# Attention inside a fused kernel: third and fourth group of transposes in one go, the fourth copy ahead of the scaling

## What is computed

```
B, H, S, D = 4, 8, 576, 64; window = 128
scores = scale * q @ k^T
scores = where(0 <= i - j < window, scores - slope_h * |i - j|, -1e9)
attn = exp(scores - max); attn = attn / (sum(attn) + 1e-9)
x = attn @ v                                   # heads side by side: B x S x 512
h = (x^T @ U @ V)^T;  u = x + h
x = u + relu(u @ w_ch1) @ w_ch2
h = relu(x @ w_in); split into u, v; v normalised, mixed over tokens by w_spatial, + b_spatial
out = (u * v) @ w_out
```

## Time and profile before

| | |
|---|---|
| median of 3 runs | 717.57 us (716.21 to 717.58) |
| the profiled execution | 718.08 us |
| its span, first to last instruction | 716.3 us |
| TensorE matmuls busy | 705.1 us, 98% |
| TensorE weight loads busy | 659.8 us, 92% |
| VectorE busy | 452.4 us, 63% |
| ScalarE busy | 339.0 us, 47% |
| GpSimd busy | 178.9 us, 25% |
| TensorE clock granted, mean | 0.998 of full |

### The profile page before, as it was taken

One profiled execution on the slowest core, in us unless ns is written; L12 is line 12 of the kernel. 1 busy time (PEld: TensorE's weight loads), 2 busy tenths in 40 slices (PEclk: granted clock), 3 DMA queues, 4 the chain that ended last, 5 costly groups with the idle time before them and its releaser, 6 DMA issues.

```text
span 716.3 us, 12975 instructions
## 1 busy us (share of the span) xinstructions
PE 705.1 (98%) x4624; PEld 659.8 (92%) x4624; DVE 452.4 (63%) x1032; ACT 339.0 (47%) x765; POOL 178.9 (25%) x183
## 2 busy tenths in 40 slices
PE   8999999999999999999999999999999999999998
PEld 5677777789999999999999999999898998998997
DVE  6979797898673274339868967976384354354341
ACT  5888788864352243234443444444352432432422
POOL 2498646510009807650050000000010100100100
PEclk9999999999999999999999999999999999999999
DMA  7659974055547856799276175468800100100101
GB/s 215 194 194 395 366 277 143 17 191 177 220 147 266 303 181 217 263 384 382 92 244 217 45 264 183 156 216 283 336 1 1 67 0 0 66 0 0 66 1 67
DMA packets 72145, 122.46 MB, mean 171 GB/s; under 512 B 4896, under 2 KB 43808, under 8 KB 71584
## 3 DMA queue, kind: packets, MB, share of 16 engines
q1 hardware_dynamic: 72096, 121.82, 49.1%
HBM read 74.29 MB, written 47.51 MB: 170 GB/s over the span
## 4 chain that ended last, share of the span: by engine, by line
PE 75%; DVE 4%; ACT 0%; issue 0%; DVEq 0%
PE bank L1917 8%; PE bank L1919 8%; PE bank L1918 8%; PE bank L1959 4%; PE bank L1961 4%; PE bank L1960 4%; PE wide L1959 3%; PE wide L1961 3%; PE wide L1960 3%; PE bank L2068 2%; PE bank L2070 2%; PE bank L2069 2%; PE bank L1884 2%; PE bank L1882 2%; PE bank L1883 2%; PE wide L1883 2%
## 5 line engine op out<-in xcount | busy, mean ns | idle before, releaser
L1917 PE MATMUL bank<-xs,w1s 128*128 128x384 f32 x336 | 113.0, 336 | 1.0 <-DVE tok L1442 0.8
L1919 PE MATMUL bank<-xs,w1s 128*128 128x384 f32 x336 | 112.3, 334 | 0.0
L1918 PE MATMUL bank<-xs,w1s 128*128 128x384 f32 x336 | 112.3, 334 | 0.0
L1075 ACT ACTIVATE rk<-tok 128x768 fp32r<-128x768 f32 x72 | 61.0, 849 | 71.3 <-PE bank L1961 32.4
L916 POOL TENSOR_TENSOR vl<-vr,vh 128x512 fp32r<-128x512 f32 x8 | 11.3, 1407 | 291.9 <-ACT vh L1200 291.9
L1053 ACT ACTIVATE sums_u<-bank 128x384 f32<-128x384 f32 x72 | 35.4, 491 | 88.7 <-PE bank L1919 88.5
L929 ACT ACTIVATE sc<-sc,mn 128x256 f32<-128x256 f32 (+1 forms) x144 | 67.0, 469 | 18.6 <-DVE mn L1260 18.4
L1959 PE MATMUL bank<-rk,w2q 128*128 128x384 f32 x208 | 69.9, 336 | 0.3 <-DVE rk L1464 0.3
L1960 PE MATMUL bank<-rk,w2q 128*128 128x384 f32 x208 | 69.5, 334 | 0.0
L1961 PE MATMUL bank<-rk,w2q 128*128 128x384 f32 x208 | 69.5, 334 | 0.0
L1917 PEld LDWEIGHTS bank<-xs,w1s 128*128 128x128 f32 x336 | 63.1, 188 | 2.7 <-issue 1.3
(11 more groups left out here) (212 smaller groups left out, 1822.1 us busy)
## 6 DMA issues: line engine op xcount, KB each, us to landing
r_scr<-tok SPq DMA_DIRECT2D x20, 768.0 KB, 3.9
tok<-r_scr SPq DMA_DIRECT2D x15, 768.0 KB, 7.1
w1raw<-w SPq DMA_DIRECT2D x32, 256.0 KB, 3.9
w2q<-w_scr SPq DMA_DIRECT2D x4, 2048.0 KB, 11.1
wc_scr<-wprep SPq DMA_DIRECT2D x12, 512.0 KB, 6.5
w_scr<-tok SPq DMA_DIRECT2D x11, 512.0 KB, 3.8
qkraw<-qk SPq DMA_DIRECT2D x16, 320.0 KB, 5.0
qkraw<-qk SPq DMA_DIRECT2D x16, 288.0 KB, 3.8
```

Of the source, the lines that this page charges most:

```text
L1075: act.activation(rk[:, n % RING, 0], raw(g, RAW_OF[m])[:, 2 * j:2 * j + 2, :], ACT.Relu if m <= 3 else ACT.Copy).then_inc(rk_hi, 1)
L1917: pe.matmul(o, wh, ah, start=(k == 0 and m in FRESH), stop=False, skip_group_check=True)
L1918: pe.matmul(o, wl, ah, start=False, stop=False, skip_group_check=True)
L1919: last = pe.matmul(o, wh, al, start=False, stop=(k == 1), skip_group_check=True)
```

## The change

On TensorE, in every pair step, the fourth group of transposes moves from behind the turning back of the earlier pair to directly behind the third group. On VectorE the copy of the fourth group moves from behind the scaling of the earlier pair to ahead of it. Nothing else changes: the same instructions with the same waits, in another order. TensorE's written-out tail stays as it was.

```diff
--- before.py
+++ after.py
@@ -1321,10 +1321,10 @@
                 score(b, i, range(0, AFTER_X))
                 if i == 2 and (whole or b >= 1):
                     lo_t(b - 1)
+                if one:
+                    keep_pt(*back(b, i, 1), 3)
                 if two:
                     normalise(*back(b, i, 2))
-                if one:
-                    keep_pt(*back(b, i, 1), 3)
                 score(b, i, range(AFTER_X, NT))
                 if whole or b >= ago:
                     add_u(b - ago, k, pt_ps)
@@ -1846,10 +1846,9 @@
                 scores_z(b, i)
                 if one:
                     turn(*back(b, i, 1), 2)
+                    turn(*back(b, i, 1), 3)
                 if two:
                     turn_back(*back(b, i, 2))
-                if one:
-                    turn(*back(b, i, 1), 3)
                 scores_y(b, i)
                 if two:
                     turn_x(*back(b, i, 2))
```

## The result

| | before | changed |
|---|---|---|
| median of 5 runs | 717.57 us (716.21 to 717.80) | 720.05 us (719.46 to 720.46) |
| span of the profiled execution | 716.3 us | 718.6 us |

The ratio is 1.0040 with a 95% interval of 1.0029 to 1.0052. The changed kernel is slower by 2.5 us; the forecast was 720.6, +3.0.

A forecast was written before the change was run, and what follows sets the result against it. TensorE was taken as the bound, its matmul row busy 705.1 of 716.3 us. Step losses 1.53 + 0.96 + 0.68 + 0.21 = 3.38, less 0.34 given back, made +3.0: 720.6 us, range 718.6 to 722.2.

The forecast's parts named there:

- the load of `qkraw`: In p = 6 (pair steps p = 4b + i) TensorE waits for this late load; up to 0.34 us given back.
- fourth pairs: p = 15, 11, 7, counted with p = 5: scaling 0.58 later less 0.40 slack, 0.17 us each, 0.68 for four.
- third pairs: p = 6, 10, 14: no slack, scaling 0.61 later, 0.10 back before the mixing; 0.51 us each, 1.53 for three.
- p = 3: Fourth pair step of batch 0: a loss of 0.21 us, lower bound 0.09.
- p = 2: Pair step of batch 0: its 0.3 us loss is taken by the next step's 1.71 wait for VectorE.
- p = 4: First pair step of batch 1: loss and the filled 0.20 us wait for `xt` cancel, 0.
- The slack: How late the scaled tile may come before TensorE's turn: 0.23 us in p = 12, 0.40 in p = 15, none in p = 14.
- Copy to scaling: VectorE, from the fourth copy's start to the scaling's start: 0.72 us taken, 0.60 as lower bound.
- First and second looped pairs: p = 8, 9, 12, 13: scaling 0.48 later less 0.23 slack, 0.24 us each, 0.96 for four.
- Only third pairs pay: Rival, attention stage: slack covers all other steps; about +1.0 us, 718.6; chance 0.15.
- Faster: Rival: the earlier copy releases TensorE sooner before each step's value products; -2.7 us, 714.9; chance 0.05.
- ScalarE caught: Rival: delayed `xh` and `tok` copies push ScalarE's exponentials in the last batch; +4.9 us, 722.5; chance 0.12.

## Why the prediction was right

The direction and the mechanism came out; the time was 0.5 us below the forecast. That the sum came so close is in part luck. Before the load of `qkraw` the forecast had 3.38, and the loss by the steps without that load was 3.09. But the fourth pairs were 0.68 too high, and third pairs (0.30), p = 3 (0.11) and p = 2 (0.06) too low; p = 4 was 0.14 too high. By its steps:

*Starting point.* Right. Time lost in TensorE's queue in attention is lost at the end: 2.38 at the stage's last turn, 2.3 in the span.

*The slack.* Right in its size in most steps. Two points of the fourth pairs confirm it: in p = 15 the scaled tile is 0.42 later against its score in the changed kernel and the turn loses 0.04; with the copy alone it is 0.96 later and the turn loses 0.58. Both leave 0.38, where the forecast had 0.40. The 0.23 is right for p = 9 and 13 but not for p = 12, from which it was worked out: there the scaled tile came 0.44 later and the turn lost 0.28, so the slack was 0.16 (p = 8 has 0.17). The forecast took 0.05 from VectorE's end to TensorE's turn, the value of p = 14; in p = 12 it is 0.12.

*Copy to scaling.* Mis-sized. I took 0.72 between their starts, from the pair L1301 and scaling, with 0.60 as the bound. The changed kernel has 0.61 in p = 4, 5, 7, 11, 15; the 0.77 and 0.78 in p = 8, 9, 12, 13 are turning back, which ends late. The copy alone shows 0.60 in these four too. In third pairs, however, the copy stands 0.72 behind L1301, and the scaling again 0.72 to 0.73 behind the copy (p = 14: 124.05, 124.77, 125.50). Each starts 0.03 or 0.04 after the end of the instruction ahead, where in p = 4, 5, 7, 11 and 15 the scaling starts 0.08 or 0.09 before the copy's end. So the 0.72 does not come with the scaling as follower, as the forecast had it; it comes with L1301, and reaches past the copy. What the Trainium skill says in VectorE: DVE Perf Modes, section The DRAIN you can't avoid, that a semaphore on each of a chain of copies adds nothing, agrees with the 0.60 to 0.61 behind the copy. What makes the two instructions behind L1301 wait 0.72 stays open. L1301 is the one of these whose operands start at partition 64 (`low` in the code); the others start at partition 0. No run here varied that.

*Third pairs.* Mechanism right, forecast 0.51 each, measured 0.60 to 0.62: the copy stands 0.72 behind L1301 and not 0.61. The 0.10 ahead of the mixing came back as foreseen. Three steps: 1.83 against 1.53.

*First and second looped pairs.* Forecast 0.24 each, measured 0.28, 0.22, 0.26, 0.21: 0.97 against 0.96. Of the sum's terms this is the closest, but two errors meet in it: the scaled tile came 0.43 to 0.45 later and not 0.48, and in p = 8 and 12 the slack was smaller. Bound by turning back (0.54 behind its last load, before and after), one of the two releasers the forecast named.

*Fourth pairs and p = 5.* Forecast 0.17 each, 0.68; measured 0.04 at the idle time and -0.04 to 0.04 from turn to turn. This is the term that was mis-sized most, the price of 0.72 taken for 0.60. The lower bound, 0.07, was nearer.

*The rest.* p = 3 0.32 (forecast 0.21). p = 4 gained 0.14 (forecast 0), with this row in place of the wait of the earlier trace rows:

```profile
36.71 0.55 PEld L1794 LDWEIGHTS wide<-ident,xt 128*128 128x128 f32 x5
```

p = 2 lost 0.20, of which 0.14 went in p = 3's wait; the forecast had all of it go there. The late `qkraw` took 0.2 in the profile (0.34 in the forecast), but as it moves between executions this term was no more than a guess.

*The rivals.* Only third pairs pay: wrong, the first and second looped pairs lose 0.97 beside them. Faster: the gap before the value products stayed at 0.16 with the copy long done; it isn't a wait for the copy. ScalarE caught: its wait for the scaled tile appears, but its delay stays inside its idle time, and the turns show no loss beyond VectorE's. The Trainium skill's Perfetto Trace Analysis, section Identifying the Most-Contended Engine, would have the most-contended engine optimised first. What that engine does was the same here (matmuls busy 705.1 and 704.7 us, weight loads 659.8 and 658.7), and 2.5 us were lost in what it waits for.

What the text had missed is the coupling that the halves show: TensorE's half needs VectorE's, else the mixing waits for the copy; VectorE's half without TensorE's costs three times the whole.

## What to carry to other kernels

When an order is changed in a queue, find the instruction whose result the busiest engine waits for, and compare its delay with the slack in each kind of step; a sum over kinds held here to 0.5 us, with single steps off by up to 0.2 both ways and some of that cancelling. Filling an engine's idle time ahead of such an instruction is only free up to the slack: 0.38 in fourth pairs, 0.16 to 0.23 in first and second, nothing in third. Two halves of a reordering on two engines have to be costed together.

## What the runs showed of the hardware that I had not expected

- Of several waits ahead of one VectorE instruction it matters which is met last: 0.54 us from the releasing engine's last load with two further waits behind it, at most 0.40 with the same wait last, in the first and second pairs of the looped batches; elsewhere 0.36 and at most 0.41.
- Behind a VectorE copy of 0.69 us the next instruction starts after 0.60 to 0.61 us, before the copy's end. With L1301 just ahead of the copy, both the copy and the scaling behind it start only after 0.72 to 0.73 us, each after the end of the one before.
- Between TensorE's weight loads with 128 and with 64 rows stands 0.17 us, and 0.33 the other way, when nothing is waited for. The value products' loads (128 rows, 64 columns) also start 0.15 to 0.17 behind loads of 128 x 128, so the number of rows is not shown to be the only cause. With turning back (whose last load has 64 columns) directly ahead, the 0.17 became 0.20 in every step of the changed kernel from p = 4 on.
- The first loads of the kernel shift everything behind them by up to 1.5 us between the profiled executions, and the wait for one late load in p = 6 varies from none to 1.0 us; differences of some tenths have to be read from step to step, not from two spans.
